# Wide block-diagonal products within a chunk, in the steps of a linear-attention recurrence that also form Gram products

## The reference

```
k_n = k / (norm(k) + 1e-6)
for t in range(768):
    y[t]   = q[t] @ state
    v_old  = k_n[t] @ state
    state += beta[t] * outer(k_n[t], v[t] - v_old)
x1 = g1(y @ w_in1) @ w_out1        # g1 = cubic / (1 + |b0 h| + |b1| h^2)
out = g2(x1 @ w_in2) @ w_out2      # g2 = h * tanh(softplus(h))
```

## Time and profile before

| | us |
|---|---|
| median of 3 runs | 1130.83 (1129.53 to 1133.27) |
| the profiled execution | 1131.52 |
| its span, first to last instruction | 1129.7 |
| its mean granted TensorE clock | 0.958 |

### The profile page before, as it was taken

How to read it: one execution, slowest core, us unless ns; L and a number is a source line. 1 busy time by engine, 2 the same in 40 slices (tenths; PEclk the granted TensorE clock), 3 DMA queues, 4 the chain that set the end, 5 groups by cost and what they waited for, 6 DMA issues and landing times.

```text
span 1129.7 us, 24251 instructions
## 1 busy us (share of the span) xinstructions
PE 1026.9 (91%) x10280; PEld 816.6 (72%) x10280; DVE 870.2 (77%) x948; ACT 779.8 (69%) x991; POOL 227.1 (20%) x380
## 2 busy tenths in 40 slices
PE   4488888888778999999999997999999999999997
PEld 3266666666667888777787876778888888888885
DVE  5966666565388888897887868999787878888885
ACT  1133444465598999989989987986776767676764
POOL 5087888880000010010010000000000000000000
PEclk7578999899989999999999999999999999999999
DMA  7823443323443333435234363430100001010000
GB/s 178 237 60 101 115 130 101 84 77 101 118 91 77 80 91 73 111 63 123 56 67 116 60 168 85 121 112 1 57 1 23 32 0 56 0 56 1 29 1 28
DMA packets 35104, 86.99 MB, mean 77 GB/s; under 512 B 4416, under 2 KB 12096, under 8 KB 35008
## 3 DMA queue, kind: packets, MB, share of 16 engines
q1 hardware_dynamic: 27584, 59.13, 17.3%
q0 software_dynamic: 6912, 25.17, 11.7%
q10 hardware_dynamic: 512, 1.31, 0.5%
HBM read 46.27 MB, written 14.16 MB: 53 GB/s over the span
## 4 chain that ended last, share of the span: by engine, by line
PE 34%; DVE 20%; ACT 12%; issue 6%; DMA 1%; ACTq 0%; DVEq 0%; POOLq 0%
PE o_ps L874 6%; PE o_ps L875 6%; PE o_ps L876 6%; PE h_ps L874 6%; PE h_ps L876 6%; PE h_ps L875 6%; DVE val L1098 5%; DVE den L1055 5%; ACT rec L962 4%; DVE pa L1061 3%; ACT rec L970 2%; DVE val L1082 2%; ACT pa L938 2%; DMA val<-pa 1%; DVE den L1089 1%
## 5 line engine op out<-in xcount | busy, mean ns | idle before, releaser
L874 PE MATMUL o_ps<-g_hi,w_hi_early 128*128 128x512 f32 x288 | 115.6, 401 | 20.8 <-DVE g_lo L1104 15.4
L951 ACT ACTIVATE g_hi<-val 128x1024 fp32r<-128x1024 f32 x96 | 102.0, 1062 | 41.8 <-DVE val L1098 36.1
L865 POOL DMA_DIRECT2D val<-pa x48 | 41.4, 862 | 424.5 <-DVE pa L1061 424.5
L874 PE MATMUL o_ps<-g_hi,w_hi_late 128*128 128x512 f32 x288 | 114.1, 396 | 10.4 <-DVE g_lo L1104 9.9
L1098 DVE SCALAR_TENSOR_TENSOR val<-den,val 128x1024 f32<-128x1024 f32 x96 | 117.4, 1222 | 5.0
L1082 DVE TENSOR_TENSOR val<-val,rec 128x1024 f32<-128x1024 f32 x96 | 117.0, 1219 | 5.5 <-DMA val<-pa 5.5
L1104 DVE SCALAR_TENSOR_TENSOR g_lo<-val,g_hi 128x1024 fp32r<-128x1024 f32 x96 | 117.7, 1226 | 2.0 <-ACT g_hi L951 2.0
L875 PE MATMUL o_ps<-g_lo,w_hi_early 128*128 128x512 f32 x288 | 113.9, 396 | 0.0
L876 PE MATMUL o_ps<-g_hi,w_lo_early 128*128 128x512 f32 x288 | 113.5, 394 | 0.0
L874 PE MATMUL h_ps<-x_hi,w_hi_early 128*128 128x512 f32 x288 | 112.3, 390 | 0.7 <-DVE x_lo L1108 0.4
L875 PE MATMUL o_ps<-g_lo,w_hi_late 128*128 128x512 f32 x288 | 112.9, 392 | 0.0
(11 more groups left out here) (114 smaller groups left out, 2175.4 us busy)
## 6 DMA issues: line engine op xcount, KB each, us to landing
val<-pa POOLq DMA_DIRECT2D x48, 512.0 KB, 4.6
w_raw<-w SPq DMA_DIRECT2D x16, 768.0 KB, 5.1
kv_run<-kv_n SPq DMA_DIRECT2D x24, 384.0 KB, 3.8
x_raw<-x_dram SPq DMA_DIRECT2D x12, 768.0 KB, 5.7
kq<-kq_t SPq DMA_DIRECT2D x44, 192.0 KB, 4.0
x_dram<-stage SPq DMA_DIRECT2D x12, 384.0 KB, 4.3
x_dram<-stage SPq DMA_DIRECT2D x6, 768.0 KB, 4.2
out<-stage SPq DMA_DIRECT2D x5, 768.0 KB, 4.1
```

Source lines behind the costliest of these rows:

```text
L874: nc.tensor.matmul(dst, hi, rhs_hi, start=first, stop=False)
L951: act_fn(g_hi[:, n % 2], val[:, n % 2], ACT.Copy, scale=-1.0).then_inc(g_hi_ready, 1)
```

## The change

In the steps with `wide(tau, c)`, `within` issues 4 products of 128x128 weights instead of 16 of 32x32. The weights are `p_blk`, a copy of p_mat spread to block-diagonal form by ScalarE (`spread_p`, two activations a step, one chunk ahead, double-buffered); the moving operand is `u_row`, u without the block mask, which VectorE makes with one operation more behind u_blk. `wide` holds for stages 0 to 2 and chunks 0 and 1 of stage 3: 28 steps. In the other steps everything is as before. The tile `k_norm` is gone: x_raw takes its place, so the norms of stage 3 are loaded, summed and rooted later in stage 0, and the first x1 load goes from the end of stage 2 to the end of stage 3.

```diff
--- before.py
+++ after.py
@@ -67,6 +67,10 @@
     return ((tau + ahead, f, c2),) if tau + ahead < T else ()
 
 
+def wide(tau, c):
+    return tau < T and len(gram_parts(tau, G2 * c + 1)) > 0
+
+
 class Weights:
 
 
@@ -130,7 +134,6 @@
 
         kq = sb("kq", [P, RING * CT, 2, G2 * V * B, C])
         kv_run = sb("kv_run", [P, CT, 2, HEADS, D])
-        k_norm = sb("k_norm", [P, CG, D])
         beta = sb("beta", [P, T, CG])
         upper = sb("upper", [P, C])
         blk_mask = sb("blk_mask", [P, B])
@@ -150,6 +153,8 @@
         w_blk = sb("w_blk", [P, 2, CG, B])
         z = sb("z", [P, G2, U, D])
         u_blk = sb("u_blk", [P, G2, U, B, D])
+        u_row = sb("u_row", [P, G2, U, D])
+        p_blk = sb("p_blk", [P, 2, HEADS, B, C])
         y_tok = sb("y_tok", [P, 2, HALVES, V * D])
         state = sb("state", [P, G2, V, B, HALVES, D])
         y_stage = hand.stage[:].rearrange("p (r g n) -> p r g n", r=HALVES, g=G2)
@@ -178,6 +183,7 @@
         nv_ready = sem("nv_ready")
         ks_done, z_ready, hz_done, ublk_ready = sem("ks_done"), sem("z_ready"), sem("hz_done"), sem("ublk_ready")
         st_done, low_ready, high_ready = sem("st_done"), sem("low_ready"), sem("high_ready")
+        urow_ready, p_ready = sem("urow_ready"), sem("p_ready")
         pads_loaded, pads_zeroed = sem("pads_loaded"), sem("pads_zeroed")
         q_done, y_done, y_copied = sem("q_done"), sem("y_done"), sem("y_copied")
         t_done, t_copied = sem("t_done"), sem("t_copied")
@@ -218,11 +224,11 @@
                 done += 2
             eng.wait_ge(step, done)
 
-        k_early = [k_norm[:], hand.stage[:, 0:CG * D].rearrange("p (n d) -> p n d", n=CG),
-                   hand.x_raw[:].rearrange("p k n -> p (k n)").rearrange("p (n d) -> p n d", n=CG)]
+        k_early = [t.rearrange("p (n d) -> p n d", n=CG)
+                   for t in (hand.x_raw[:].rearrange("p k n -> p (k n)"), hand.stage[:, 0:CG * D])]
 
         def k_of(j):
-            return k_early[j] if j < RING else k_norm[:]
+            return k_early[1 if j == 1 else 0]
 
         def norm_slot(j):
             return (j, 16) if j < RING else (0, 16 * (j - RING + 2))
@@ -242,8 +248,8 @@
         @block.sync
         def _(sp):
             def load_norm(j):
-                if j >= RING:
-                    sp.wait_ge(sumsq_ready, 1 if j == RING else j)
+                if j >= 2:
+                    sp.wait_ge(sumsq_ready, 1 if j == 2 else j)
                 sp.dma_start(k_of(j).rearrange("p (c h) d -> p c (h d)", c=CT),
                              kv_n[j].rearrange("p (c a n) -> p c a n", c=CT, a=2)[:, :, 0, :]
                              ).then_inc(k_norm_loaded[norm_slot(j)[0]], 16)
@@ -280,7 +286,6 @@
             for c in range(CT):
                 load_kv(0, c)
             load_norm(2)
-            load_norm(3)
             sp.wait_ge(pads_zeroed, 4)
             for c in range(CT):
                 for r in range(HALVES):
@@ -291,7 +296,7 @@
                 if tau == T - 1:
                     for i in range(2, NP // 2):
                         w.load(sp, w1, i)
-                if tau and tau + 3 < T:
+                if tau + 3 < T:
                     load_norm(tau + 3)
                 for c in range(CT):
                     if tau + RING < T:
@@ -307,7 +312,8 @@
                         store_y(tau - 1, 1)
                     if c == 2:
                         store_y(tau, 0)
-                if tau == 2:
+                if tau == 3:
+                    sp.wait_ge(sumsq_ready, T)
                     for cp in range(2):
                         sp.wait_ge(hand.y_stored[cp], 16 + 16)
                     hand.load_x(sp, x1, 0)
@@ -438,11 +444,20 @@
             def within(tau, c, g):
                 q = index(tau, c, g)
                 pe.wait_ge(q_done, q + 1)
+                if wide(tau, c):
+                    pe.wait_ge(p_ready, CT * tau + c + 1)
+                    pe.wait_ge(urow_ready, q + 1)
                 by_event()
                 for v in range(V):
                     for r in range(HALVES):
+                        at = D * (HALVES * v + r)
+                        if wide(tau, c):
+                            last = nc.tensor.matmul(y_bank[g][:, at:at + D],
+                                                    p_blk[:, c % 2, U * g + V * r + v].rearrange("p b t -> p (b t)"),
+                                                    u_row[:, g, V * r + v],
+                                                    start=False, stop=True, skip_group_check=True)
+                            continue
                         for b in range(B):
-                            at = D * (HALVES * v + r)
                             last = nc.tensor.matmul(y_bank[g][quad(b), at:at + D],
                                                     p_mat[quad(b), tau % RING, HEADS * c + U * g + V * r + v],
                                                     u_blk[quad(b), g, V * r + v, b],
@@ -533,6 +548,18 @@
                 act.wait_ge(st_done, index(tau, c, g) + 1)
                 nc.scalar.activation(state[rows(1), g, :, :, 1], st_ps[g][rows(1)], ACT.Copy).then_inc(high_ready, 1)
 
+            def spread_p(tau, c, half):
+
+                if half == 0:
+                    act.wait_ge(gram_used, 4 * tau + 2 * (c // 2) + 2)
+                    if tau or c >= 2:
+                        act.wait_ge(y_done, index(tau, c, 0) - 2)
+                for b in (2 * half, 2 * half + 1):
+                    last = nc.scalar.activation(p_blk[:, c % 2, :, b], p_mat[:, tau % RING, HEADS * c:HEADS * c + HEADS],
+                                                ACT.Copy, scale=blk_mask[:, b:b + 1])
+                if half:
+                    last.then_inc(p_ready, 1)
+
             def copy_turned(q):
                 tau, c, g = q // NQ, q % NQ // G2, q % G2
                 if c % 2 == 0 and g == 0:
@@ -558,6 +585,9 @@
             for g in range(G2):
                 scale_v(0, 0, g)
             split = {(T - 2, 1): 0, (T - 2, 5): 1, (T - 1, 1): 2, (T - 1, 5): 3}
+            act.wait_ge(masks_loaded, 32)
+            for half in range(2):
+                spread_p(0, 0, half)
             for tau in range(T):
                 for s in range(NQ):
                     c, g = s // G2, s % G2
@@ -572,9 +602,13 @@
                         scale_v(tau, c + 1, g)
                     elif tau + 1 < T:
                         scale_v(tau + 1, 0, g)
-                    if s == 1 and tau + 3 < T:
+                    if c + 1 < CT and wide(tau, c + 1):
+                        spread_p(tau, c + 1, g)
+                    if c + 1 == CT and wide(tau + 1, 0):
+                        spread_p(tau + 1, 0, g)
+                    if s == (1 if tau else 3) and tau + 3 < T:
                         squares(tau + 3)
-                    if s == 3 and tau + 3 < T:
+                    if s == (3 if tau else 6) and tau + 3 < T:
                         roots(tau + 3)
                     if (tau, s) in split:
                         w.split_hi(nc, act, split[(tau, s)])
@@ -628,6 +662,9 @@
 
                 cp, r = f // 2, f % 2
                 dve.wait_ge(gram_done, 4 * j + f + 1)
+                if r == 0 and j >= RING:
+
+                    dve.wait_ge(p_ready, CT * (j - RING) + 2 * cp + 2)
                 if f == 0 and j:
 
                     dve.wait_ge(n_turned_ready, TURNS * j)
@@ -688,6 +725,9 @@
                 cg = HEADS * c + U * g
                 dve_tt(u_blk[:, g], hz_ps[:, 0:U * D].rearrange("p (u d) -> p u d", u=U).unsqueeze(2).broadcast_to([P, U, B, D]),
                        w_blk[:, tau % 2, cg:cg + U].unsqueeze(3).broadcast_to([P, U, B, D]), ALU.mult).then_inc(ublk_ready, 1)
+                if wide(tau, c):
+                    dve_tt(u_row[:, g], hz_ps[:, 0:U * D].rearrange("p (u d) -> p u d", u=U),
+                           wgt[:, tau, cg:cg + U].unsqueeze(2).broadcast_to([P, U, D]), ALU.mult).then_inc(urow_ready, 1)
 
             def copy_low(tau, c, g):
 
@@ -729,7 +769,6 @@
                         residual(tau, (s + 1) // G2, (s + 1) % G2)
                     elif tau + 1 < T:
                         residual(tau + 1, 0, 0)
-                    fill = s - (1 if tau == 0 else 0)
                     if (tau, s) == (0, 1):
                         root_inverse(2)
                     if (tau, s) == (0, 1):
@@ -737,19 +776,21 @@
                     if (tau, s) == (0, 7):
                         turn_n(2, 0, half_k)
                         turn_n(2, half_k, C)
+                    if (tau, s) == (0, 7):
+                        root_inverse(3)
                     if s == (7 if tau == 0 else 5) and tau + 3 < T:
                         weights(tau + 3)
                     for j, f, c2 in gram_parts(tau, s):
                         if c2 == 1:
                             scale_gram(j, f)
-                    if s == (5 if tau == 0 else 4) and tau + 3 < T:
+                    if tau and s == 4 and tau + 3 < T:
```

(4 more changed lines are left out.)

## The result

| | before | after |
|---|---|---|
| median (20 runs each) | 1131.63 us | 1140.14 us |
| lowest to highest | 1125.54 to 1135.89 | 1130.87 to 1148.15 |
| the profiled execution | 1131.52 | 1138.29 |
| its span | 1129.7 | 1135.5 |
| its mean granted clock | 0.958 | 0.950 |

The ratio after to before is 1.0070, 95% interval 1.0049 to 1.0091: slower by 0.7%, some 8 us. The forecast was 1133; the time lies at rival 4 (1139). Runs more than 1.5% above the fastest of their kernel are left out of every ratio: one of the changed kernel's 20, one of 12 in experiment 10, and three of 12 in experiment 7, the profiled one among them.

The account below looks back on a forecast made before the run. TensorE, short of instructions at packet edges, was taken to bound the first 28 steps. The terms 18.5 - 15.5 + 1.6 + 0.8 - 1.5 - 2 gave +1.9 us on 1131.5, forecast 1133, range 1122 to 1144.

Parts of the forecast that it names:

- rival 4: VectorE waits at the squares' steps and stage 0's end lower the clock at three places: +7 us, 1139; chance 0.17.
- the likeliest case: The forecast itself for the whole kernel: 1133 us, own range 1129 to 1138; chance 0.43.
- What bounds: In the first 28 steps TensorE, busy 85%, is on the path and eats instructions faster than packets bring them.
- rival 1: Instruction supply was the whole story: gaps vanish, clock stays up; -10.6 us at the end, half way about 1126; chance 0.22.
- Wide products, +18.5: Within a chunk, 8 full-width pairs replace 32 narrow ones: 0.66 us more in each of 28 steps, +18.5 us.
- Instructions, -15.5: 24 pairs fewer a step shrink TensorE's issue gaps from 22 us to 6.5 us in the 28 steps: -15.5 us.
- Rival 3: Issue gaps shrink only with the number of packets: slower by 15.7 us, 1146; chance 0.10.
- p_blk on ScalarE, +1.6: Two copies, 0.82 us a step, are covered except ahead of the squares in step 1 of two stages: +1.6 us.
- Clock, -2: In the 28 steps less standing of TensorE gives some granted clock back: -2 us, between -8 and +4.
- Places where TensorE waits anyway, -1.5: Before the Gram products of three stages TensorE's waits for VectorE hide the longer wide group: -1.5 us.
- u_row, norms, moved loads: u_row on VectorE costs nothing; stage 3's later norms cost +0.8 us at stage 0's end; moved loads taken as 0.
- The sum: All terms over the whole kernel: +1.9 us on 1131.5, the two large ones nearly cancelling.

Follow-up runs that it names:

- experiment 10: The changed kernel with each norm's sums in one piece in step 2, and wide products in all 48 steps; ratio to the kernel before 1.0026.
- experiment 7: The changed kernel with p_blk filled once at the start and no copies in the steps (stale weights, wrong y); ratio to the kernel before 1.0026.
- b_drop12: The kernel before with 12 of the 16 products within a chunk left out in the 28 steps (y wrong); ratio to the kernel before 0.9981.
- a_sums2: The changed kernel with the sums of a norm in one piece in step 2, not split over steps 1 and 2; ratio to the kernel before 0.9993.
- a_warm: The changed kernel with 32 idle products of 128 columns ahead of the update in step 2 of stages 1 and 2; ratio to the kernel before 1.0009.
- b_norms: The kernel before with only the norm part of the change, products within a chunk still narrow, nothing spread; ratio to the kernel before 1.0013.
- a_narrow: The changed kernel with all its additions (p_blk, u_row, norms) but the old 16 narrow products in all steps; ratio to the kernel before 1.0034.

## Why the prediction was right, and where it was not

The time lies in the range, but not in the forecast's own range (1129 to 1138): the likeliest case was the wrong one, one term was too small by two thirds, and one had the wrong sign. Rival 4 is what happened. That its 1139 is so close is in part luck: it had three places at 2 to 3 us, and it was two at 3 to 4. Step by step:

- **What bounds.** Right for the 28 steps: TensorE, and in it the supply of instructions. Incomplete beyond them: GpSimd's chain of inverses ends within a few us of TensorE's need for it. b_drop12 (11.34 us of waiting) and a_sums2 (0.95) show it. It took nothing from the change, because the change won nothing, and it was absent from bounds and rivals; rival 1's gain would have met it.
- **Wide products, +18.5.** The group measured 1.02 us from loads to next loads (0.98 predicted): 28 x 0.70 = 19.6. With the 0.10 that L411 gives back, the undisturbed step is 0.59 longer, 16.5 us in all. Loads 0.11 us apart, as the bounds asked; the drain behind them 0.05, not 0.1.
- **Instructions, -15.5.** Measured 22 - 4.9 = -17. Right in mechanism; the packets' number fell by five as forecast. It was right to let the longer step count here: b_drop12, with the same pairs gone and short steps, kept 13.5 us of gaps. The Trainium skill (Runtime: NRT & Kernel Launch, Instruction fetch mechanics) has the crossing of a block mostly hidden: the runs disagree, for with 3420 products instead of 4077 the gaps fell by 17 us in this stretch. Rival 3 fell with it.
- **p_blk on ScalarE, +1.6: the term that failed.** The copies took 0.89 us a pair (0.82 predicted), and they do go ahead of the squares. But the step priced only the copies' own length. TensorE's wait went to 2.88 us in both stages (1.39 in one before), +4.4 by these rows, of which the copies are 0.80 a time (experiment 7). In stage 1 of before the issue gap of 1.94 us stood in the wait's place, and the change took that gap away: a cover was lost that the sum had not named.
- **Clock, -2: wrong sign.** "Less standing should give some back" held for the issue gaps: the kernel before has spells of lower clock behind its gaps of 2.88 us (81.37), 1.94 (117.37) and 1.72 (202.76), and the changed kernel has none there. But it stands 2.88 us at two new places, and the clock fell behind these (granted 0.79 and 0.68), for longer. By the means, 0.11 and 0.13 missing at the two levels' difference of 0.5, TensorE was at the lower level for 34 of 153 us before and 41 of 159 after. That is rival 4, as it was described: two of its three places, and a_warm prices them together at some 7 us. At the third, the end of stage 0, TensorE stands 3.08 us, but the clock there is much as before (0.73 from 102 to 107 us, 0.78 before). The spells do not come in every execution: the two fastest of the changed kernel's 20 runs took 1130.87 and 1131.21 us, at a mean clock of 0.962 and 0.959.
- **Places where TensorE waits anyway, -1.5.** The three waits ahead of the Gram products (0.86, 0.20 and 0.44 us) are gone, as priced.
- **u_row, norms, moved loads.** u_row is 0.35 us and z still waited for TensorE in 24 steps. For the norms 0.8 us was allowed; TensorE stands 2.0 us longer ahead of the burst of stage 0 (3.08 for 1.12), while the time of the whole is within the noise (b_norms). Nothing shifts after the 28th step.
- **The sum.** By the rows 16.5 - 17 + 4.4 - 1.5 + 2.0 = +4.4. Issue gaps at two lines that the sum leaves out fell by 3.4 us more (update and q_state: 2.8 and 2.7 before, 1.1 and 1.0 after), so it is +1.0, and the profile's +5.7 leaves some 5 for the clock. That is an estimate from one pair of executions: the two new spells less what the old ones cost. The price of the new ones alone, some 7 us, rests on a_warm's ratio, whose interval is 0.2% to each side, and on stages 1 and 2 of its profile. What stays open: in stage 0 the spell at 1.2 GHz lasted longer in the profile of after than in that of before:

```profile
68.86 1.94 PE L455 MATMUL y_bank<-u_row,p_blk 128*128 128x48 f32 x8
```

At 1.94 us a wide group costs nearly double there; in the kernel before the clock was back by 67 us. The spell's length differs from profile to profile, also among kernels that are the same up to this place, and no run here tells whether the change has a part in it. How much of b_drop12's gain is lost to the clock, beyond GpSimd's 3 us, is open as well.

## What to carry to other kernels

When a product is made wider to save instructions, price its loads against the gaps they remove, and try the middle width first: here 128-wide weights cancelled their gain, and 64-wide ones stood 0.2% lower in both pairs, which is within the noise of each. Before an engine off the path gets 1 us more work, look at the one place in a stage where the path waits for it: 0.9 us of ScalarE, together with what else came late there, turned 1.4 us of TensorE standing into 2.9, and the lower clock behind two such places cost 7 us. And ask which engine is second: GpSimd's chain ended 2.2 us ahead of TensorE's need, so a larger gain before it could not have reached the end whole.

## What the runs showed that was not expected

- A standstill of 2.88 us was followed by a spell at 1.2 GHz (at 125.79 us the double Gram group takes 1.93 us); with 1.95 us of idle products in the same gap (a_warm) it was not. A standstill of 1.39 us (stage 2 of before) had no such spell behind it; one of 1.94 us had a short one. But one of 2.67 us (a_narrow, 164.51) had none either, so the length alone does not decide it. The ratios are 1.0009 with the idle products and 1.0070 without.
- Beside a single VectorE operation on 1536 columns, a GpSimd operation that takes 0.6 us elsewhere takes 2.44, on the chain that bounds the last stage (b_drop12). The profiles of before, after, b_drop12 and a_sums2 have two such VectorE operations each in the recurrence's second half, and each of the eight has one GpSimd operation of 2.0 to 2.5 us beside it:

```profile
240.09 2.44 POOL L214 TENSOR_TENSOR inv_t<-n_turned,inv 128x240 f32<-128x240 f32 x1
240.33 1.74 DVE L100 TENSOR_TENSOR w_lo_early<-w_raw,w_hi_early 128x1536 fp32r<-128x1536 f32 x1
```
